# Attention's matmuls on four 64x64 tiles of TensorE, and each period's products in two halves

## The chip, the cores and the metric

The kernel runs on one core of one Trainium2 chip. The metric is the device time of one execution in microseconds; three executions are taken and their median is quoted.

## What is computed

Three layers follow one another. The first is attention inside chunks of 64 tokens, over 4 batches, 8 heads, 576 positions and 64 elements a head. The second is a gated layer from 512 to 1536 columns and back, the third a layer from 512 to 2048 and back with a rational function between. All arrays are float32.

```python
scores = scale * np.matmul(q_c, k_c.transpose(0, 1, 2, 4, 3))   # chunks of 64 by 64
attn = np.exp(scores - np.max(scores, axis=-1, keepdims=True))
attn = attn / (np.sum(attn, axis=-1, keepdims=True) + 1e-09)
x = np.matmul(attn, v_c)                  # then x becomes 2304 tokens by 512
x = ((x @ w_a) * (x @ w_b)) @ w_out
h = x @ w_in
g = (a0 + a1*h + a2*h*h + a3*h*h*h) / (1 + |b0|*|h| + |b1|*h*h + 1e-06)
out = g @ w_out2
```

## The kernel before

Every engine has its own hand-written program, and semaphores tie them together. The 2304 tokens are 18 units of 128 tokens, and 6 tiles of 384 tokens (3 units each). A unit holds two chunks (`cc`) and eight heads, which stand as four pairs (`r`) of two heads (`h`).

**Attention of a unit** passes five stages, one a period, so that five units are under way at once. In stage 0 TensorE (PE in the profile) transposes q and k (L515, four transposes each into the banks `QT` and `KT`) and ScalarE (ACT) copies them out (L823, L824). In stage 1 PE makes the scores: 16 matmuls of 64 rows by 64 columns with 64 moving columns (L539), all into the bank `SC`. They use two of the four 64x64 quarters of the array: head 0 has rows and columns 0 to 63, head 1 rows and columns 64 to 127. VectorE (DVE) takes the maximum (L1083) and subtracts it (L1085), ACT takes the exponential (L837), and DVE sums (L1090), adds 1e-9 (L1092), inverts (L1094) and multiplies (L1098). In stage 2 PE transposes the result into the bank `AT` (L515) and ACT copies it in two halves of 64 partitions into `attnT` (L832), whose off-diagonal blocks stay zero. In stage 3 PE multiplies with v: 8 matmuls of 128 rows by 64 columns with 128 moving columns (L557), half of which multiply the zeros, into the bank `XP`. ACT rounds x out of that bank (`x_hi`, L841) and DVE takes the rest (`x_lo`, L1076). The float32 matmuls of stages 1 and 3 are two records each in the trace, each with a weight load of its own; a transpose is one.

**The lead** is the first five units (`LEAD`), with transposes of the identity between the stages to keep PE busy. **The merged stage** follows: 15 periods, three to a tile for the first five tiles. Each has the attention stages of five units and then 24 matmuls with 384 moving columns. In the first two periods of a tile they are the products a and b of one step (`merged_block` with `r < G1`): ACT copies b out (L892), DVE multiplies a with it (L1112), ACT rounds that (`g_hi`, L894) and DVE takes the rest (`g_lo`, L1115). In the third period they are the four sums of the down product, which ACT copies out (L900). Late in the stage ACT also rounds operands for what comes next (`round_t` at L881, `round_w` at L863), two behind each of several periods, and GpSimd (POOL) makes the sums they come from. All that ACT and DVE do stands in one fixed order per engine: an instruction whose wait is not over holds up those behind it.

**The rest**, from 157.8 us on, is the gated layer's other columns (L643, L596) and the third layer.

The order of a period on PE before is: transposes of q; product with v; transposes of k; transposes of the attention of the unit before; scores; 24 products.

Of the kernel before, what the change touches and what calls it, by code (L numbers as in the profile page):

```python
# [20 lines left out]
def attention_moe_moe2(nc, q, k, v, w_a, w_b, w_out1, w_in, w_out2, a, b, out):  # L21
# [63 lines left out]
    with ExitStack() as ctx:  # L85
# [63 lines left out]
        attnT = tmp[:, 4 * D:6 * D].rearrange("p (r h n) -> p r h n", r=HP, h=2)  # L149

        def grouped(x):
            return x.rearrange("p (g k) -> p g k", k=CH)

        def spread(x):
            return x[:, 0:8].unsqueeze(2).to_broadcast([P, 8, CH])

        QT, KT, SC, AT, XP = range(3, 8)
# [240 lines left out]
        def _(pool):  # L398
            nc.gpsimd.memset(ident[:], 0.0).then_inc(consts_ready, 1)
            nc.gpsimd.memset(attnT, 0.0).then_inc(consts_ready, 1)  # L400
            nc.gpsimd.memset(bias_ln[:], QC * 2.0 ** -SHIFT).then_inc(consts_ready, 1)
            nc.gpsimd.memset(bias_exp[:], -SHIFT * math.log(2.0)).then_inc(consts_ready, 1)
            pool.wait_ge(consts_ready, 4)
# [103 lines left out]
        def _(pe):  # L507
# [10 lines left out]
            def attention(turn, slot, stages):  # L518
# [3 lines left out]
                lead = isinstance(i, int) and i < LEAD  # L522
# [5 lines left out]
                def wait_scores():  # L528
                    pe.wait_ge(qkT_copied, 2 * i)
                    if 2 in stages:  # L530
                        pe.wait_ge(sub_done, i - 1)

                def scores():
                    for r in range(HP):
                        for cc in range(2):
                            at = slice((2 * r + cc) * CH, (2 * r + cc + 1) * CH)
                            for h in range(2):
                                rows = slice(h * HD, (h + 1) * HD)
                                last = nc.tensor.matmul(ps[rows, SC, at], qT[rows, at], kT[rows, at], start=True, stop=True)  # L539
                    last.then_inc(scores_done, 1)  # L540

                def transpose_attn():
                    pe.wait_ge(attn_done, i - 1)
                    if 3 in stages:
                        pe.wait_ge(attnT_copied, 2 * (i - 2))
                    transposes(AT, attn).then_inc(attnT_done, 1)

                def times_v():
                    v_turn, v_slot = before(turn, slot, 3)
                    pe.wait_ge(attnT_copied, 2 * (i - 2))  # L550
# [26 lines left out]
                else:  # L577
# [3 lines left out]
                    if 3 in stages:  # L581
                        times_v()
                    if 0 in stages:
                        transposes(KT, qk_raw(slot)[1]).then_inc(qkT_done, 1)
                    if 1 in stages:
                        wait_scores()
                    if 2 in stages:
                        transpose_attn()
                    if 1 in stages:
                        scores()  # L590
# [18 lines left out]
            def first1(kk):  # L609

                t, f = kk // G1, kk % G1
                if kk == PLAIN:
                    pe.wait_ge(x_ready, UNITS)
                    pe.wait_ge(part_copied, DC * MERGED)
# [4 lines left out]
                tok = slice(t * TILE, (t + 1) * TILE)  # L619
                for m in range(2):  # L620
                    last = product3(ps[:, 2 * (kk % 2) + m, 0:TILE],
                                    [(w_cols(2 * m * PW + c * G1 * P + f * P), both(x_hi, x_lo, c, tok))
                                     for c in range(DC)])
# [70 lines left out]
            def merged_block(t, r, last=False):  # L694

                if r < G1:
                    if r == 0:
                        pe.wait_ge(x_ready, UPT * t + UPT)
                        pe.wait_ge(part_copied, DC * t + 1)
                    pe.wait_ge(product_done, G1 * t + r + 1)  # L700
                    tok = bass.ds(t * TILE, TILE)
                    for m in range(2):
                        last = product3(ps[:, m, 0:TILE],
                                        [(w_cols(2 * m * PW + c * G1 * P + r * P), both(x_hi, x_lo, c, tok))
                                         for c in range(DC)])
                    last.then_inc(ab_done, 1)
                else:
                    pe.wait_ge(w_ready, FIRSTS)
                    pe.wait_ge(g_ready, G1 * t + G1)
                    for c in range(DC):  # L710
                        if last and c == 2:
                            attention(*LAST, {3, 4})
                        if c in (0, DC - 1):
                            pe.wait_ge(part_copied, DC * t + (1 if c == 0 else 2))
                        product3(ps[:, (2, 0, 1, 2)[c], 0:TILE],
                                 [(w_cols(4 * PW + f * D + c * P), both(g_hi, g_lo, 1 + f))
                                  for f in range(G1)]).then_inc(part_done, 1)
# [52 lines left out]
            pe.wait_ge(consts_ready, 5)  # L770
# [8 lines left out]
            for r, stages in enumerate(({0, 1, 2, 3, 4}, {1, 2, 3, 4}, {2, 3, 4})):  # L779
# [543 lines left out]
```

## Time and profile before

| | before |
|---|---|
| median of 3 executions | 911.8 us (911.66 to 912.16) |
| profiled execution | 911.71 us, its span 909.9 us |
| PE busy | 898.4 us, 99% of the span |
| DVE, ACT, POOL busy | 673.1, 515.4, 364.9 us |
| granted clock of TensorE | full in all 40 slices |

The span runs from the first to the last instruction of the program; 1.8 us of the execution lie around it. A busy share is an average over the whole span, and the merged stage is 126 us of it, so that stage is read by itself below. The engines' lines are numbered by the code above.

### The profile page before, as it was taken

Reading aid. Unit: us, or ns where it says so; the run is one execution under the profiler, and the core shown is the slowest. Engines: PE = TensorE matmul, PEld = TensorE weight load, DVE = VectorE, ACT = ScalarE, POOL = GpSimd, SP = SyncE. Lnnn points to the kernel's source line nnn. Section 1 sums busy time; section 2 is a strip of 40 time slices with the busy share of each in tenths; the row PEclk is TensorE's granted clock in tenths of the full one; section 3 lists DMA queues with packets and bytes.
Section 4 is the critical chain, followed back from the end, with each engine's and each line's share of the span. In section 5 each row is a group of like instructions: output and inputs, shape, how many; then the busy total and the mean of one; then the engine's idle time right before and its main releaser. Section 6 shows DMA issues by size and latency. Waiting matters only on the chain.

```text
span 909.9 us, 14077 instructions
## 1 busy us (share of the span) xinstructions
PE 898.4 (99%) x5596; PEld 849.3 (93%) x5596; DVE 673.1 (74%) x874; ACT 515.4 (57%) x787; POOL 364.9 (40%) x302
## 2 busy tenths in 40 slices
PE   8999999899999999999999999999999999999998
PEld 8898999899999999999999998999999999999996
DVE  3657553666666667656565799997999999989987
ACT  4655674344444444445554587886667566666562
POOL 2109133577887778888976023210111011100000
PEclk9999999999999999999999999999999999999999
DMA  9865310222222222223211020002000200000102
GB/s 206 177 151 106 83 24 25 82 70 70 70 68 70 70 65 77 68 82 98 71 44 57 13 93 1 1 1 93 1 1 0 92 2 1 1 1 29 42 36 104
DMA packets 103234, 53.35 MB, mean 59 GB/s; under 512 B 58880, under 2 KB 94720, under 8 KB 103168
## 3 DMA queue, kind: packets, MB, share of 16 engines
q1 hardware_dynamic: 103168, 52.45, 21.6%
q8 instruction: 44, 0.72, 0.3%
q14 instruction: 22, 0.18, 0.1%
HBM read 47.71 MB, written 4.72 MB: 58 GB/s over the span
## 4 chain that ended last, share of the span: by engine, by line
PE 92%; DVE 4%; ACT 2%; issue 1%; POOL 0%; DVEq 0%; ACTq 0%; POOLq 0%
PE ps L596 40%; PE ps L643 23%; PE ps L764 19%; PE ps L515 3%; PE ps L539 2%; PE ps L557 2%; PE ps L511 1%; DVE tmp L1267 1%; DVE tmp L1273 1%; ACT w L1041 1%; PE ps L632 0%; ACT g_hi L1054 0%; ACT tmp L1027 0%; ACT tmp L1024 0%; DVE tmp L1263 0%
## 5 line engine op out<-in xcount | busy, mean ns | idle before, releaser
L596 PE MATMUL ps<-x_hi,w 128*128 128x384 f32 x960 | 255.3, 337 | 0.6 <-DVE tmp L1286 0.3
L596 PEld LDWEIGHTS ps<-x_hi,w 128*128 128x128 f32 x960 | 174.4, 188 | 3.6 <-DVE tmp L1286 0.7
L764 PE MATMUL ps<-w,g_hi 128*128 128x512 f32 x576 | 177.5, 391 | 0.0
L596 PE MATMUL ps<-x_lo,w 128*128 128x384 f32 x480 | 160.8, 335 | 0.0
L596 PE MATMUL ps<-g_hi,w 128*128 128x384 f32 x560 | 148.7, 335 | 1.0 <-issue 1.0
L439 POOL TENSOR_TENSOR w<-w 128x512 fp32r<-128x512 f32 x32 | 47.0, 1476 | 231.8 <-ACT w L876 231.8
L643 PE MATMUL ps<-x_hi,w 128*128 128x384 f32 x480 | 134.0, 334 | 1.5 <-DVE tmp L1150 1.5
L764 PEld LDWEIGHTS ps<-w,g_hi 128*128 128x128 f32 x576 | 107.4, 188 | 21.0 <-ACT g_hi L1054 0.4
L764 PE MATMUL ps<-w,g_lo 128*128 128x512 f32 x288 | 112.1, 392 | 0.0
L1140 DVE TENSOR_TENSOR y<-y,ps 128x384 f32<-128x384 f32 x120 | 65.6, 552 | 58.6 <-PE ps L596 58.6
L643 PE MATMUL ps<-w 128*128 128x384 f32 x540 | 103.4, 334 | 1.2 <-ACT ps L935 1.2
L596 PEld LDWEIGHTS ps<-g_hi,w 128*128 128x128 f32 x560 | 101.7, 188 | 1.8 <-issue 1.4
L955 ACT CAST g_hi<-tmp 128x384 fp32r<-128x384 f32 x60 | 30.8, 514 | 116.4 <-DVE tmp L1155 90.5
L643 PEld LDWEIGHTS ps<-w 128*128 128x128 f32 x540 | 94.4, 188 | 1.5 <-ACT ps L935 1.5
L596 PE MATMUL ps<-g_lo,w 128*128 128x384 f32 x280 | 93.6, 334 | 0.0
L596 PEld LDWEIGHTS ps<-x_lo,w 128*128 128x128 f32 x480 | 90.1, 188 | 1.7
L643 PEld LDWEIGHTS ps<-x_hi,w 128*128 128x128 f32 x480 | 87.8, 188 | 1.8 <-DVE tmp L1150 1.8
L429 POOL TENSOR_TENSOR w<-w 128x512 fp32r<-128x512 f32 (+1 forms) x48 | 72.5, 1538 | 20.8 <-ACT w L863 19.7
L643 PE MATMUL ps<-x_lo,w 128*128 128x384 f32 x240 | 80.2, 334 | 0.0
L1041 ACT ACTIVATE w<-tmp,bias_ln 128x768 f32<-128x768 f32 x48 | 45.1, 940 | 61.8 <-DVE tmp L1273 61.5
L1024 ACT ACTIVATE tmp<-ps 128x768 f32<-128x768 f32 x48 | 39.0, 813 | 65.6 <-PE ps L596 65.6
L1267 DVE SCALAR_TENSOR_TENSOR tmp<-tmp,coef 128x768 f32<-128x768 f32 x48 | 52.7, 1098 | 28.5 <-ACT tmp L1027 28.4
(113 smaller groups left out, 1590.7 us busy)
## 6 DMA issues: line engine op xcount, KB each, us to landing
w<-in_moe_w_out SPq DMA_DIRECT2D x32, 256.0 KB, 3.0
out<-y SPq DMA_DIRECT2D x18, 256.0 KB, 2.0
y<-in_q SPq DMA_DIRECT2D x16, 256.0 KB, 4.4
y<-in_k SPq DMA_DIRECT2D x16, 256.0 KB, 4.9
y<-in_v SPq DMA_DIRECT2D x16, 256.0 KB, 3.2
w<-in_moe_w_a SPq DMA_DIRECT2D x16, 256.0 KB, 3.0
w<-in_moe_w_b SPq DMA_DIRECT2D x16, 256.0 KB, 3.6
w<-in_moe_w_in SPq DMA_DIRECT2D x16, 256.0 KB, 3.9
```

The lines of the kernel that those rows point to most:

```text
L429: nc.gpsimd.tensor_tensor(w[:, w_slot(n), LO, at:to], raw_w(n, at, to), w[:, w_slot(n), HI, at:to], ALU.subtract).then_inc(ws_ready, 1)
L439: nc.gpsimd.tensor_tensor(w2_at(w, fp, LO, i), w2_at(w32, fp, LO, i), w2_at(w, fp, HI, i), ALU.subtract).then_inc(w2_ready, 1)
L515: last = nc.tensor.transpose(ps[:, bank, r * P:(r + 1) * P], x[:, r * P:(r + 1) * P], ident[:])
L539: last = nc.tensor.matmul(ps[rows, SC, at], qT[rows, at], kT[rows, at], start=True, stop=True)
L596: last = nc.tensor.matmul(dst, left, right, start=n == 0, stop=n == 3 * len(pairs) - 1)
L643: last = nc.tensor.matmul(ps[:, bank, 0:TILE], left, moving, start=i == 0 and not onto, stop=i == 5, skip_group_check=onto)
L764: last = nc.tensor.matmul(out_bank(n), left[:, 2 * (m % 2) + e, u * P:(u + 1) * P], w[:, slot2(fp), right, DC * HALF + e * D:DC * HALF + ( ...
L955: nc.scalar.copy(g_hi[:, 2 * ti + n % 2, :], corner[:, 2 * (n % 2) + 1 - ti, :]).then_inc(g_hi_done, 1)
L1024: nc.scalar.activation(habs, h, ACT.Abs).then_inc(habs_done, 1)
L1041: nc.scalar.activation(rec, den3[m % 2], ACT.Ln, scale=2.0 ** -SHIFT, bias=bias_ln[:, 0:1]).then_inc(ln_done, 1)
L1140: nc.vector.tensor_tensor(y[:, t, at], y[:, t, at], ps[:, 4 + c, 0:TILE], ALU.add).then_inc(y_added, 1)
L1267: nc.vector.scalar_tensor_tensor(out=den[cur], in0=den[cur], scalar=coef[:, 6:7], in1=habs, op0=ALU.add, op1=ALU.mult).then_inc(den_done, 1)
```

## The change

Scores and products with v both become 16 matmuls of 64 rows by 64 columns with 64 moving columns, spread over all four 64x64 quarters of the array. `attnT` no longer holds zeros, and ACT copies it at once (L895 of the changed kernel in place of two of L832). Scores and x share two banks: scores stand in the upper half of the columns of banks 6 and 7, x in the lower half (in the lead x stands in banks 1 and 2). For that sharing PE waits for `x_ready` ahead of the scores and for `sub_done` ahead of the product with v. A period on PE becomes: product with v; transposes of q and k; 12 products; scores; transposes of attention; 12 products. On DVE the product a times b moves in between the sum and the addition of 1e-9 of the attention. On ACT the copy of attention moves behind those of k and q, and the rounding of a product moves to the next period, behind that of x.

```diff
-        attnT = tmp[:, 4 * D:6 * D].rearrange("p (r h n) -> p r h n", r=HP, h=2)
+        attnT = tmp[:, 4 * D:5 * D].rearrange("p (r s n) -> p r s n", r=HP, s=2)
...
-        QT, KT, SC, AT, XP = range(3, 8)
+        QT, KT, AT, SC = 3, 4, 5, 6
+        raw_scores = ps[:, SC:SC + 2, D // 2:D].rearrange("p c (r k) -> p c r k", k=CH)
+        def x_bank(i):
+            return 1 if i < LEAD else SC
+        def raw_x(i):
+            return ps[:, x_bank(i):x_bank(i) + 2, 0:D // 2].rearrange("p c (r q) -> p r c q", q=CH)
...
                     if 2 in stages:
                         pe.wait_ge(sub_done, i - 1)
+                    if not lead:
+                        pe.wait_ge(x_ready, i - 2)
                 def scores():
...
                             for h in range(2):
-                                rows = slice(h * HD, (h + 1) * HD)
-                                last = nc.tensor.matmul(ps[rows, SC, at], qT[rows, at], kT[rows, at], start=True, stop=True)
+                                rows, half = slice(h * HD, (h + 1) * HD), h ^ cc
+                                to = slice(D // 2 + r * CH, D // 2 + (r + 1) * CH)
+                                last = nc.tensor.matmul(ps[half * CH:(half + 1) * CH, SC + cc, to],
+                                                        qT[rows, at], kT[rows, at], start=True, stop=True)
...
+                    if not lead:
+                        pe.wait_ge(sub_done, min(i - 1, UNITS))
                     vs = v_raw(v_slot)
                     for r in range(HP):
-                        for h in range(2):
-                            last = nc.tensor.matmul(ps[h * HD:(h + 1) * HD, XP, r * P:(r + 1) * P],
-                                                    vs[:, (2 * r + h) * HD:(2 * r + h + 1) * HD],
-                                                    attnT[:, r, h, :], start=True, stop=True)
+                        for cc in range(2):
+                            rows = slice(cc * CH, (cc + 1) * CH)
+                            for h in range(2):
+                                last = nc.tensor.matmul(ps[h * HD:(h + 1) * HD, x_bank(i) + cc, r * CH:(r + 1) * CH],
+                                                        vs[rows, (2 * r + h) * HD:(2 * r + h + 1) * HD],
+                                                        attnT[rows, r, h ^ cc, :], start=True, stop=True)
...
+            def first_half(t, f, m):
+                if m == 0:
+                    if f == 0:
+                        pe.wait_ge(x_hi_done, UPT * t + UPT)
+                        pe.wait_ge(part_copied, DC * t + 1)
+                    pe.wait_ge(product_done, G1 * t + f + 1)
+                    product_hi(ps[:, 0, 0:TILE], first_operands(t, f, 0))
+                    if f == 0:
+                        pe.wait_ge(x_ready, UPT * t + UPT)
+                    product_lo(ps[:, 0, 0:TILE], first_operands(t, f, 0))
+                else:
+                    product3(ps[:, 1, 0:TILE], first_operands(t, f, 1)).then_inc(ab_done, 1)
+            def part_half(t, cs):
+                if cs[0] == 0:
+                    pe.wait_ge(w_ready, FIRSTS)
+                for f in range(G1):
+                    pe.wait_ge(g_ready, G1 * t + f + 1)
+                    for c in cs:
+                        if f == 0 and c == 1:
+                            pe.wait_ge(product_done, G1 * (t + 1) + 1)
+                        part_sum(t, f, c)
...
             for j in range(MERGED // 2):
                 for r in range(2 * RING):
-                    attention(2 * j + (LEAD + r) // RING, (LEAD + r) % RING, {0, 1, 2, 3, 4})
-                    merged_block(2 * j + r // UPT, r % UPT)
+                    for half in range(2):
+                        attention(2 * j + (LEAD + r) // RING, (LEAD + r) % RING, {0, 1, 2, 3, 4}, half)
+                        merged_half(2 * j + r // UPT, r % UPT, half)
...
+            def merged(turn, slot, stages, t, r):
+                attention(turn, slot, stages, 0)
+                if r > 0:
+                    first_g(G1 * t + r - 1)
+                if r == G1:
+                    copy_part(t, 0)
+                    copy_part(t, 1)
+                attention(turn, slot, stages, 1)
                 if r < G1:
+                    copy_b(G1 * t + r)
+                elif t < MERGED - 1:
+                    copy_part(t, 2)
+                    copy_part(t, 3)
```

On PE, in the second period of a tile, the attention's instructions stood in one piece ahead of the products (`ident,y` is a transpose of q or k, `ident,tmp` one of attention; the 24 products are L596):

```order
L515 MATMUL ps<-ident,y 128x128 [waits qkT_copied,qk_loaded0]
L515 MATMUL ps<-ident,y 128x128 x3
L557 MATMUL ps<-tmp,y 64x128 [waits x_ready,v_loaded0,attnT_copied]
L557 MATMUL ps<-tmp,y 64x128 x7
L515 MATMUL ps<-ident,y 128x128 x4
L515 MATMUL ps<-ident,tmp 128x128 [waits attn_done,attnT_copied,sub_done,qkT_copied]
L515 MATMUL ps<-ident,tmp 128x128 x3
L539 MATMUL ps<-tmp 64x64 x16
L596 MATMUL ps<-x_hi,w 128x384 [waits product_done]
L596 MATMUL ps<-x_lo,w 128x384
```

Now they stand in two pieces, with twelve products behind each (the first twelve begin at L616, the second at L628; L580 is the product with v, L557 the scores):

```order
L580 MATMUL ps<-tmp,y 64x64 [waits x_ready,sub_done,v_loaded0,attnT_copied]
L580 MATMUL ps<-tmp,y 64x64 x15
L530 MATMUL ps<-ident,y 128x128 [waits qkT_copied,qk_loaded0]
L530 MATMUL ps<-ident,y 128x128 x7
L616 MATMUL ps<-x_hi,w 128x384 [waits product_done]
L617 MATMUL ps<-x_hi,w 128x384
...
L621 MATMUL ps<-x_lo,w 128x384 x4
L557 MATMUL ps<-tmp 64x64 [waits x_ready,sub_done,qkT_copied]
L557 MATMUL ps<-tmp 64x64 x15
L530 MATMUL ps<-ident,tmp 128x128 [waits attnT_copied,attn_done]
L530 MATMUL ps<-ident,tmp 128x128 x3
L628 MATMUL ps<-x_hi,w 128x384
...
L580 MATMUL ps<-tmp,y 64x64 [waits x_ready,sub_done,v_loaded1,attnT_copied]
```

The product with v has moved ahead of the transposes of q, the scores ahead of those of attention and behind twelve products, and both have a wait more (`sub_done`, `x_ready`).

On DVE, from the sum of the exponentials in the same kind of period to the rest of x, the order was:

```order
L1090 TENSOR_REDUCE ssum<-tmp 128x8 [waits exp_done]
L1092 TENSOR_SCALAR ssum<-ssum 128x8 [waits sum_done]
L1094 RECIPROCAL sinv<-ssum 128x8 [waits eps_done]
L1098 TENSOR_TENSOR tmp<-tmp,sinv 128x512 [waits attnT_done,inv_done]
L1112 TENSOR_TENSOR tmp<-ps,tmp 128x384 [waits b_copied]
L1115 TENSOR_TENSOR g_lo<-tmp,g_hi 128x384 [waits g_hi_done]
L1076 TENSOR_TENSOR x_lo<-ps,x_hi 128x4x128 [waits x_hi_done]
```

and it is now:

```order
L1166 TENSOR_REDUCE ssum<-tmp 128x8 [waits exp_done]
L1187 TENSOR_TENSOR tmp<-ps,tmp 128x384 [waits b_copied]
L1170 TENSOR_SCALAR ssum<-ssum 128x8 [waits sum_done]
L1172 RECIPROCAL sinv<-ssum 128x8 [waits eps_done]
L1176 TENSOR_TENSOR tmp<-tmp,sinv 128x2x4x64 [waits attnT_done,inv_done]
L1192 TENSOR_TENSOR g_lo<-tmp,g_hi 128x384 [waits g_hi_done]
L1153 TENSOR_TENSOR x_lo<-ps,x_hi 128x4x128 [waits x_hi_done]
```

The product of a and b (`tmp<-ps,tmp`) has moved ahead of three small instructions and of the multiplication that the transposes of attention wait for.

On ACT, around the two roundings of `round_t` behind the first of three periods (`w<-w`), the order was:

```order
L892 COPY tmp<-ps 128x384 [waits ab_done]
L894 CAST g_hi<-tmp 128x384 [waits product_done]
L881 CAST w<-w 128x768 [waits t_made] x2
L841 CAST x_hi<-ps 128x4x128 [waits av_done]
L832 COPY tmp<-ps 64x8x64 [waits av_done,attnT_done]
L832 COPY tmp<-ps 64x8x64
L823 COPY tmp<-ps 128x512 [waits scores_done,qkT_done]
```

and it is now:

```order
L953 COPY tmp<-ps 128x384 [waits ab_done]
L944 CAST w<-w 128x768 [waits t_made] x2
L903 CAST x_hi<-ps 128x4x128 [waits av_done]
L957 CAST g_hi<-tmp 128x384 [waits product_done]
L888 COPY tmp<-ps 128x512 [waits scores_done,qkT_done]
L889 COPY tmp<-ps 128x512
L895 COPY tmp<-ps 128x512 [waits av_done,attnT_done]
```

The roundings stood behind `g_hi`; they now stand ahead of it and of x's rounding, because `g_hi` has moved to the next period.

## Rows read from the trace of the kernel before

**Rows 1.** The page's table of engines: busy us, share, instructions.

```profile
PE 898.4 (99%) x5596; PEld 849.3 (93%) x5596; DVE 673.1 (74%) x874; ACT 515.4 (57%) x787; POOL 364.9 (40%) x302
```

**Rows 2.** Windows by stage: PE, PEld, DVE, ACT, POOL busy us, PEclk, DMA.

```profile
31.68:157.83 126.15, 124.73 (x1233) 115.38 (x1229) 70.49 (x123) 73.47 (x138) 40.29 (x30) 1.00 0.39 85
```

**Rows 3.** Timeline of PE, one period: start us, length us, line, form, records.

```profile
103.83 0.45 PE L596 MATMUL ps<-x_hi,w 128*128 128x384 f32 x1
104.11 0.34 PE L596 MATMUL ps<-x_lo,w 128*128 128x384 f32 x1
...
108.13 0.60 PE L515 MATMUL ps<-ident,y 128*128 128x128 f32 x4
108.66 1.09 PE L557 MATMUL ps<-tmp,y 128*64 128x128 f32 x16
109.68 0.66 PE L515 MATMUL ps<-ident,y 128*128 128x128 f32 x4
...
110.71 1.15 PE L539 MATMUL ps<-tmp 64*64 64x64 f32 x32
111.78 0.45 PE L596 MATMUL ps<-x_hi,w 128*128 128x384 f32 x1
```

**Rows 4.** Lines L539 and L557: duration ns min/median/max of one record.

```profile
L539 PE MATMUL ps<-tmp x576: 218/218/268, 10.8 to 134.7; 64*64 64x64 f32 x192
...
L557 PE MATMUL ps<-tmp,y x288: 272/273/323, 19.9 to 145.0; 128*64 128x128 f32 x144
```

**Rows 5.** PE and its loads, product with v to 68.40, scores to 70.42 us.

```profile
68.29 0.33 PE L557 MATMUL ps<-tmp,y 128*64 128x128 f32 x2
...
68.29 0.20 PEld L557 LDWEIGHTS ps<-tmp,y 128*64 128x64 f32 x4 [0.17 <-issue]
...
70.34 0.27 PE L539 MATMUL ps<-tmp 64*64 64x64 f32 x2
...
70.34 0.19 PEld L539 LDWEIGHTS ps<-tmp 64*64 64x64 f32 x4 [0.17 <-issue]
```

**Rows 6.** Timeline of ACT behind the products that end at 108.13 us.

```profile
108.33 0.48 ACT L892 COPY tmp<-ps 128x384 f32<-128x384 f32 x1 [2.30 <-PE ps L596]
109.43 0.51 ACT L894 CAST g_hi<-tmp 128x384 fp32r<-128x384 f32 x1 [0.62 <-DVE tmp L1112]
109.85 1.56 ACT L881 CAST w<-w 128x768 fp32r<-128x768 f32 x2
111.31 0.58 ACT L841 CAST x_hi<-ps 128x512 fp32r<-128x512 f32 x1
```

**Rows 7.** Timeline of DVE in the same stretch.

```profile
107.23 0.69 DVE L1098 TENSOR_TENSOR tmp<-tmp,sinv 128x512 f32<-128x512 f32 x1
108.84 0.56 DVE L1112 TENSOR_TENSOR tmp<-ps,tmp 128x384 f32<-128x384 f32 x1 [0.92 <-ACT tmp L892]
109.97 0.56 DVE L1115 TENSOR_TENSOR g_lo<-tmp,g_hi 128x384 fp32r<-128x384 f32 x1 [0.58 <-ACT g_hi L894]
111.92 0.69 DVE L1076 TENSOR_TENSOR x_lo<-ps,x_hi 128x512 fp32r<-128x512 f32 x1 [1.39 <-ACT x_hi L841]
```

**Rows 8.** Timeline of PE: the two places where it stands still.

```profile
78.36 0.63 PE L515 MATMUL ps<-ident,tmp 128*128 128x128 f32 x4 [0.43 <-DVE tmp L1098]
...
140.30 0.66 PE L515 MATMUL ps<-ident,tmp 128*128 128x128 f32 x4
141.94 0.41 PE L596 MATMUL ps<-g_hi,w 128*128 128x384 f32 x1 [0.99 <-issue]
```

**Rows 9.** Timeline of DVE ahead of the first of them.

```profile
75.96 2.14 DVE L1098 TENSOR_TENSOR tmp<-tmp,sinv 128x512 f32<-128x512 f32 x1
```

**Rows 10.** Timeline of ACT: roundings of weights behind the sums.

```profile
124.71 1.14 ACT L863 CAST w<-w 128x512 fp32r<-128x512 f32 x2
```

**Rows 11.** Timeline of PE in the lead.

```profile
18.77 1.15 PE L539 MATMUL ps<-tmp 64*64 64x64 f32 x32
19.85 1.09 PE L557 MATMUL ps<-tmp,y 128*64 128x128 f32 x16
```

More of the change, by code:

```diff
@@ L516, in transposes, with attention @@
                 return last
-            def attention(turn, slot, stages):
+            def attention(turn, slot, stages, part=0):
                 i = turn * RING + slot
-                lead = isinstance(i, int) and i < LEAD
+                lead = i < LEAD
                 def wait_qk():
@@ L618, in first1 @@
                     pe.wait_ge(product_done, kk)
-                tok = slice(t * TILE, (t + 1) * TILE)
                 for m in range(2):
-                    last = product3(ps[:, 2 * (kk % 2) + m, 0:TILE],
-                                    [(w_cols(2 * m * PW + c * G1 * P + f * P), both(x_hi, x_lo, c, tok))
-                                     for c in range(DC)])
+                    a_b = ps[:, 2 * (kk % 2) + m, 0:TILE]
+                    if kk == PLAIN:
+                        pe.wait_ge(part_copied, DC * MERGED - 1 + m)
+                        product_hi(a_b, first_operands(t, f, m))
+                        if m == 0:
+                            pe.wait_ge(x_ready, UNITS)
+                        last = product_lo(a_b, first_operands(t, f, m))
+                    else:
+                        last = product3(a_b, first_operands(t, f, m))
                 last.then_inc(ab_done, 1)
@@ L692, in second_sum @@
                               for fi in range(G1)]).then_inc(sum_done1, 1)
-            def merged_block(t, r, last=False):
-                if r < G1:
[L697 to L706, printed above, removed]
-                else:
[L708 to L717, printed above, removed]
@@ new lines, in first_operands @@
+            def first_operands(t, f, m):
+                return [(w_cols(2 * m * PW + c * G1 * P + f * P), both(x_hi, x_lo, c, slice(t * TILE, (t + 1) * TILE)))
+                        for c in range(DC)]
+            def first_half(t, f, m):
+                if m == 0:
+                    if f == 0:
[6 more added lines that the diff above has]
+                    product_lo(ps[:, 0, 0:TILE], first_operands(t, f, 0))
+                else:
+                    product3(ps[:, 1, 0:TILE], first_operands(t, f, 1)).then_inc(ab_done, 1)
@@ new lines, in part_bank, with part_sum @@
+            def part_bank(c):
+                return ps[:, (2, 0, 1, 2)[c], 0:TILE]
+            def part_sum(t, f, c):
+                if f == 0 and c in (0, DC - 1):
+                    pe.wait_ge(part_copied, DC * t + (1 if c == 0 else 2))
+                at = 4 * PW + f * D + c * P
+                for left, right in ((HI, g_hi), (LO, g_hi), (HI, g_lo)):
+                    last = nc.tensor.matmul(part_bank(c), first_w(left, at, P), right[:, 1 + f, :],
+                                            start=f == 0 and (left, right) == (HI, g_hi), stop=f == G1 - 1 and right is g_lo)
+                if f == G1 - 1:
+                    last.then_inc(part_done, 1)
@@ L809, in _, with attention @@
         def _(act):
-            def attention(turn, slot, stages):
+            def attention(turn, slot, stages, part=0):
                 i = turn * RING + slot
@@ L1068, in _, with attention @@
         def _(dve):
-            def attention(turn, slot, stages):
+            def attention(turn, slot, stages, s=None):
                 i = turn * RING + slot
-                lead = isinstance(i, int) and i < LEAD
+                lead = i < LEAD
                 def rest_x():
                     dve.wait_ge(x_hi_done, i - 2)
-                    at = bass.ds((i - 3) * P, P)
-                    nc.vector.tensor_tensor(x_lo[:, :, at], ps[:, XP, :].rearrange("p (c n) -> p c n", c=DC),
-                                            x_hi[:, :, at], ALU.subtract).then_inc(x_ready, 1)
+                    nc.vector.tensor_tensor(x_unit(x_lo, i - 3), raw_x(i), x_unit(x_hi, i - 3), ALU.subtract).then_inc(x_ready, 1)
                 if 3 in stages and not lead:
@@ L1103, in _, with product1 @@
             dve.wait_ge(part_copied, 1)
[L1104 to L1107 removed]
+            def product1(s, a_bank, slot, same_slot=False):
                 dve.wait_ge(b_copied, s + 1)
```

139 lines of the change are left out of this document (81 added, 58 removed).

## The prediction

> **What bounds the kernel now.** The page's table of engines comes first: PE is busy 99% of the span, its weight loads 93%, DVE 74%, ACT and POOL less [rows 1]. So time is won by taking work off PE and lost by making it wait, and the question is whether four quarters of the array do the same matmuls in less time than two. The change touches the lead and the merged stage alone. A window over the merged stage shows PE busy for 124.73 of 126.15 us, at full clock [rows 2]; busy PE is not PE at its peak, so I read one period in the timeline [rows 3]. It takes 111.78 - 103.83 = 7.95 us: 24 products 4.30, transposes of q 0.53, product with v 1.02, eight transposes 1.03, scores 1.07. These follow without a hole, and 13 of the 15 periods look like this. PE stands still at two places, for 0.43 us until DVE's L1098 is done, and at 141.94, where the sums wait for `g_lo` [rows 8]. The four transposes ahead of the second begin at 140.30 and need 0.5 as elsewhere, so that wait is 141.94 - 140.80 = 1.1 us. The first comes from one DVE instruction of 2.14 us [rows 9] that takes 0.69 elsewhere [rows 7].
>
> **What four tiles can give.** The trace has scores on two quarters, head 0 in one, head 1 in the diagonally opposite one, in turn. They share no rows and no columns. If quarters worked side by side, the two heads' matmuls would show it already. 16 scores are 32 records and the last is 0.218 long [rows 3, 4], so they start over 1.15 - 0.22 = 0.93 us, 0.058 per matmul of two records. The product with v has 16 records over 1.09 - 0.27 = 0.82 us; eight matmuls of 128 moving columns, at a pitch of 0.109. In the first 0.08 us of the scores (to 70.42) four weight loads have started, those of both heads, but only two matmul records, the two of one matmul; the other head's begin after it. In the first 0.11 us of the product with v (to 68.40) it is the same [rows 5]. So I find pairs of records of one matmul under way together and no overlap of one quarter with another. And 0.058 for 64 columns against 0.109 for 128 says that halving the moving columns just about halves the time: as the product with v also doubles its matmuls, from 8 to 16, it gains nothing. I take both groups at the pitch of the scores.
>
> The Trainium skill speaks for the change here: TensorEngine Tiling (Array Packing), section Key Properties, has different tiles load weights and multiply in parallel. By that rule each group would need half the slots; this trace's two quarters don't show it, so in the sum it has no place, but it is a rival.
>
> **The sum, part by part.**
> - Scores: the same 32 records of the same form, 0.
> - Product with v: 32 records as the scores', 1.07 to 1.08, in place of 1.02 [rows 3]: +0.054 for each of 18 units, +1.0. Bounds: -0.41 each if pairs overlap (below), and +0.2 each if neighbours on the same rows got in each other's way, as far as no row shows them.
> - Changes of shape: four in a period before and after. What differs is what stands behind the scores. Before, it is a product: the second follows the first after 0.28 us [rows 3], where (4.30 - 0.11) / 24 = 0.17 is usual, 0.11 lost. After, it is transposes, which behind the product with v take 0.66 for four instead of 0.60 [rows 3], 0.06 lost. 15 x -0.05 = -0.7. In the lead the product with v follows the scores 1.08 us after their start [rows 11], a change of shape between; afterwards both have one shape: -0.1 for two units and, as ACT copies attention at once and PE waits for that copy at the lead's end, some 0.1 more. I take -0.3; if q and k land too late for it, 0.
> - Waits that go: 0.43 and 1.1 [rows 8], -1.5. Their covers now are the twelve products ahead of the transposes of attention, and the half of the sums that needs only the first `g`.
> - Waits that come, since on ACT and DVE the order is other. Let Z be the end of a period's products on PE (108.13 in rows 3). ACT copies b at Z+0.20 for 0.48 [rows 6]. PE starts the product with v at Z+0.09, transposes from Z+1.17, and the first twelve matmuls at Z+2.10. Behind the copy of b ACT now has, in three periods, the two roundings of 0.83 with 0.73 from one start to the next [rows 6], before it comes to x and `g_hi`: x starts at Z + 0.20 + 0.39 + 2 x 0.73 = Z+2.05 (0.39 is the copy's 0.48 less the 0.09 by which neighbours overlap), `g_hi` at Z+2.54, done Z+3.05; `g_lo` on DVE, 0.56 [rows 7], done Z+3.65. If the next period is one of sums, PE needs it after six matmuls, Z + 2.10 + 6 x 0.173 = Z+3.14: wait 0.6. One period later ACT rounds two pieces of w in 1.14 [rows 10] between the sums' copies and x: x done Z + 0.20 + 0.39 + 1.06 + 0.58 = Z+2.23, seen at 2.30, wanted at 2.10: 0.2.
> - In the last two periods PE has no q and k to transpose and comes 0.93 earlier. Bank 0 must be free: copy of b, then the product a times b, 0.56 [rows 7], done at Z+1.30; PE is there at Z+1.17: 0.15. Then the scores wait for `x_ready`: with two roundings (0.73 and 0.53) x starts at Z+1.85, `g_hi` at 2.34, `g_lo` from 2.88, x_lo at 3.35 for 0.69 [rows 7], seen Z+4.1; PE is there at 1.33 + 2.19 + 0.09 = Z+3.6: 0.5. In the last period `g_lo` waits behind DVE's small instructions and the 0.69 of attention: product done Z+1.25, multiplication Z+2.3, `g_lo` Z+2.95 against PE at Z+2.3: 0.65. And while POOL works and DVE's instructions stretch as in [rows 9], I allow 0.3 once, ahead of the scores. Together 0.6 + 0.2 + 0.15 + 0.5 + 0.65 + 0.3 = +2.4.
>
> The order of the other periods costs nothing. Where ACT has no roundings, x is rounded once the product with v is done, by Z+1.85, and `g_lo` (Z+2.9) and x_lo (Z+3.5) come before the scores at Z + 2.10 + 2.08 + 0.09 = Z+4.27. That cover is 0.7 us thick, and what stands behind the scores would be late by whatever eats through it. SP's loads wait for the same semaphores at much the same times, and the rest of the kernel starts later by the sum.
>
> Sum: 1.0 - 0.7 - 0.3 - 1.5 + 2.4 = +0.9. The profiled execution took 911.71 us, its span of 909.9 and 1.8 around it, which is 0.1 below the median; on it the sum gives 912.6, on the median 912.7. I say **912.6 us**, no change that could be told: a measurement of this kernel can tell about 0.2%, 1.8 us, from none.
>
> **Rivals.**
> - *Quarters do work side by side*, because head 0 and head 1 both wrote the bank `SC` before and now matmuls that follow one another use two banks. The Trainium skill, same page, section Gotcha 1: PSUM Pressure, says that different row tiles can't access the same PSUM bank at the same time; no run here shows whether that is what kept them apart. Then 16 matmuls need 8 slots of 0.058: -0.47 for the scores and 1.02 - 0.61 = -0.41 for the product with v, -15.8 over 18 units. PE then comes 0.47 earlier to each of its waits: five waits grow by that and the sums of four tiles get one of 0.3, +3.5 beside the 0.9 of the other terms less the 1.0 for v. Result 911.7 - 15.8 + 3.5 - 0.1 = about 899; if only every second pair overlaps, about 904. For it: the pairs of records that do start together. Against: two banks don't help head 0 and head 1, which are neighbours and still share one. Chance 0.24.
> - *A dearer DVE chain, slower.* Product a times b now stands ahead of attention's last four steps, and the rest of x behind them must be done before the scores. It decides once copy of b to x_lo is longer than the cover of 0.7. One instruction stretched by 1.45 [rows 7, 9] costs 0.7. If four or five periods had one, +3 to +4: 916. POOL is busy 40.29 of 126.15 us of the stage [rows 2], and only one of these long ones shows before. Chance 0.09, with anything like it on the v matmuls.
> - *The new waits are smaller than worked out*, with the rest as forecast: 910.5 to 911.5, still no difference. It is part of the forecast's 0.67.
>
> **How the numbers follow.** Forecast with its own range of 911 to 914.5: 0.67. Of it I put 0.03 below 910.0 and 0.11 above 913.6, the bounds of 0.2%. With 0.24 for the first rival: faster 0.27. With 0.09 for the second: slower 0.21, and 0.52 for the same. Leaving out 2 in 10 takes the range down into the first rival: 900 to 915.
>
> **What would show it.** Right: 32 records of the product with v spread over 0.93 us, a period of 7.95, waits of about 0.6 at the sums near 118 us and again near 142, and about 0.5 ahead of the scores near 135. Wrong: records of either group closer than 0.029 on average, so a group shorter than 1 us and periods near 7.1 (first rival), or idle PE ahead of the scores in most periods behind `x_lo` (second). If the shape changes cost other than 0.05 a period, the end of the merged stage tells: it was 157.83 and should be 158.7.

## The result and the profile after

The changed kernel takes **920.11 us** (median of 5 runs, 917.85 to 922.66) against 911.8 before: ratio 1.0089, 95% interval 1.0076 to 1.0102. It is 0.9% slower, and outside the range of 900 to 915. The profiled execution is the slowest of the five, 922.66 us with a span of 919.6. The first product of the part behind the merged stage starts at 167.43 us, where it was 157.83: all of the loss is ahead of it.

The page's table of engines and its row of the granted clock, against [rows 1]:

```profile
PE 892.9 (97%) x5884; PEld 840.8 (91%) x5884; DVE 683.4 (74%) x874; ACT 502.9 (55%) x769; POOL 364.0 (40%) x301
...
PEclk9998989999999999999999999999999999999999
```

PE is busy 5.5 us less and its span is 9.7 longer, so it waits. One period in the timeline of PE, against [rows 3]:

```profile
101.18 0.42 PE L616 MATMUL ps<-x_hi,w 128*128 128x384 f32 x1
...
103.47 0.69 PE L557 MATMUL ps<-tmp 64*64 64x64 f32 x32
104.09 0.66 PE L530 MATMUL ps<-ident,tmp 128*128 128x128 f32 x4
...
106.78 0.69 PE L580 MATMUL ps<-tmp,y 64*64 64x64 f32 x32
107.40 1.09 PE L530 MATMUL ps<-ident,y 128*128 128x128 f32 x8
108.25 0.42 PE L616 MATMUL ps<-x_hi,w 128*128 128x384 f32 x1
```

The period is 108.25 - 101.18 = 7.07 us, where it was 7.95. The scores take 0.69 in place of 1.15 and the product with v 0.69 in place of 1.09; less the last record's 0.22, 32 records start over 0.47. The four quarters do give what the first rival said. Where it is lost again, the waits of PE over the merged stage tell (engine, line, what it waited for, us, times, longest):

```profile
PE ps L755 <- DVE g_lo L1192: 8.4, 3, 3.8
PE ps L557 <- DVE x_lo L1153: 5.3, 2, 2.8
PE ps L616 <- DVE tmp L1187: 0.5, 1, 0.5
PE ps L616 <- ACT x_hi L903: 0.4, 1, 0.4
```

Five waits of 1.5 to 3.8 us, each for the last instructions of DVE's chain. The groups of DVE in the same stretch (busy us, mean ns of one) show which of them is late:

```profile
L1176 DVE TENSOR_TENSOR tmp<-tmp,sinv 128x512 f32<-128x512 f32 x14 | 18.1, 1292 | 0.5
L1192 DVE TENSOR_TENSOR g_lo<-tmp,g_hi 128x384 fp32r<-128x384 f32 x10 | 11.4, 1136 | 0.0
...
L1166 DVE TENSOR_REDUCE ssum<-tmp 128x8 f32<-128x512 f32 x14 | 9.6, 686 | 10.6 <-ACT tmp L899 10.6
L1187 DVE TENSOR_TENSOR tmp<-ps,tmp 128x384 f32<-128x384 f32 x10 | 5.6, 558 | 6.2 <-ACT tmp L953 6.2
```

The multiplication (L1176) has a median of 0.69 and a longest of 2.27; `g_lo` (L1192) goes from 0.55 to 2.15. The sum over the exponentials (L1166) and the product of a and b (L1187) keep their 0.69 and 0.56. The timeline of all engines at the first stall names the partner:

```profile
64.39 1.83 POOL L460 TENSOR_TENSOR x_lo<-x_hi,x_lo 128x768 f32<-128x768 f32 x1 [32.44 <-PE ps L628]
...
65.34 0.91 DVE L1170 TENSOR_SCALAR ssum<-ssum 128x8 f32<-128x8 f32 x1
65.72 0.60 PE L755 MATMUL ps<-g_hi,w 128*128 128x384 f32 x2
...
66.30 1.81 POOL L462 TENSOR_TENSOR w<-x_lo,x_hi 128x768 f32<-128x768 f32 x1
66.34 0.52 PE L755 MATMUL ps<-g_hi,w 128*128 128x384 f32 x2
66.52 2.14 DVE L1176 TENSOR_TENSOR tmp<-tmp,sinv 128x512 f32<-128x512 f32 x1
66.69 0.34 PE L755 MATMUL ps<-g_lo,w 128*128 128x384 f32 x1
...
68.19 2.13 POOL L464 TENSOR_TENSOR w<-w,x_lo 128x768 f32<-128x768 f32 x1
68.58 2.15 DVE L1192 TENSOR_TENSOR g_lo<-tmp,g_hi 128x384 fp32r<-128x384 f32 x1
70.28 2.14 POOL L468 TENSOR_TENSOR w<-x_hi,x_lo 128x768 f32<-128x768 f32 x1
70.66 0.68 DVE L1153 TENSOR_TENSOR x_lo<-ps,x_hi 128x512 fp32r<-128x512 f32 x1
70.79 1.01 PE L755 MATMUL ps<-g_hi,w 128*128 128x384 f32 x2 [3.76 <-DVE g_lo L1192]
```

POOL's instruction ends at 66.30 + 1.81 = 68.11; the multiplication, 0.69 by itself, ends 0.55 later, so nearly all of its work comes behind POOL's. POOL's next one starts ahead of that end and takes 2.13 in place of 1.83, and `g_lo` waits for it in turn. `x_lo`, of which one input is in PSUM, starts beside a POOL instruction and takes its 0.68. The two that make PE late have both inputs in SBUF. This is what the Trainium skill states (SBUF — State Buffer, section Who interferes with whom): a DVE instruction with two SBUF inputs contends with a GpSimd (here POOL) instruction that reads SBUF, and the second to issue waits for all of the first. The trace agrees, but for the first 0.14 us of the multiplication's 0.69. Two inputs in SBUF are not the only case: the small addition of 1e-9 (L1170), with one input of 8 columns in SBUF, takes 0.91 here beside POOL's instruction of 64.39, and 0.16 elsewhere. What decides for that one no run separates.

A second loss stands behind the wait. Windows of the same trace (stretch, us, busy us of PE, PEld, DVE, ACT, POOL, then the granted clock):

```profile
31.00:66.00 35.00, 35.00 (x499) 31.54 (x498) 20.93 (x39) 18.84 (x37) 2.56 (x3) 1.00 0.69 155
66.00:70.80 4.80, 1.04 (x7) 0.71 (x5) 4.73 (x5) 0.00 (x1) 4.64 (x4) 0.88 0.72 164
70.80:75.00 4.20, 4.20 (x43) 3.65 (x44) 1.29 (x3) 1.69 (x4) 4.12 (x3) 0.50 0.00 0
75.00:77.90 2.90, 2.90 (x16) 2.65 (x15) 2.10 (x3) 1.79 (x4) 2.82 (x2) 0.74 0.00 0
```

PE was idle for 3.76 us, and for the 4.2 us behind it the granted clock is 0.50, the level of 1.2 GHz, and 0.74 on average in the 2.9 us after that: two products take 1.01 us where they took 0.60 at full clock (65.72 above).

### The profile page after: what moved, and what is told of

It is laid out like the page before. It is cut to its first block, busy times and chain, and to the rows that moved or that the text cites. A ratio compares the mean times of both kernels' runs of the same rounds, so it can differ in the third digit from the quotient of the medians.

```text
span 919.6 us, 14651 instructions
## 1 busy us (share of the span) xinstructions
PE 892.9 (97%) x5884; PEld 840.8 (91%) x5884; DVE 683.4 (74%) x874; ACT 502.9 (55%) x769; POOL 364.0 (40%) x301
## 4 chain that ended last, share of the span: by engine, by line
PE 86%; DVE 7%; ACT 3%; SPq 2%; issue 1%; DMA 1%; DVEq 0%; ACTq 0%
PE ps L628 35%; PE ps L679 23%; PE ps L821 19%; PE ps L530 2%; PE ps L755 2%; DVE tmp L1176 1%; SPq L313 1%; PE ps L557 1%; DVE tmp L1350 1%; DVE g_lo L1192 1%; PE ps L621 1%; PE ps L616 1%; DVE tmp L1356 1%; PE ps L617 1%; PE ps L580 1%
## 5 line engine op out<-in xcount | busy, mean ns | idle before, releaser
L628 PE MATMUL ps<-x_hi,w 128*128 128x384 f32 x864 | 232.5, 339 | 0.5 <-DVE tmp L1369 0.3
L628 PEld LDWEIGHTS ps<-x_hi,w 128*128 128x128 f32 x864 | 158.8, 190 | 2.9 <-DVE tmp L1369 0.7
L628 PE MATMUL ps<-x_lo,w 128*128 128x384 f32 x432 | 145.7, 337 | 0.0
L679 PE MATMUL ps<-x_hi,w 128*128 128x384 f32 x480 | 133.9, 334 | 1.4 <-DVE tmp L1232 1.4
L628 PE MATMUL ps<-g_hi,w 128*128 128x384 f32 x480 | 126.5, 334 | 0.0
L679 PEld LDWEIGHTS ps<-x_hi,w 128*128 128x128 f32 x480 | 87.7, 188 | 1.8 <-DVE tmp L1232 1.8
L628 PEld LDWEIGHTS ps<-g_hi,w 128*128 128x128 f32 x480 | 87.0, 188 | 0.0
L628 PEld LDWEIGHTS ps<-x_lo,w 128*128 128x128 f32 x432 | 82.0, 190 | 1.7
L679 PE MATMUL ps<-x_lo,w 128*128 128x384 f32 x240 | 80.2, 334 | 0.0
L628 PE MATMUL ps<-g_lo,w 128*128 128x384 f32 x240 | 80.2, 334 | 0.0
```

What stands on the lines that cost most here:

```text
L628: last = nc.tensor.matmul(dst, left, right, start=n == 0, stop=n == 3 * len(pairs) - 1)
L679: last = nc.tensor.matmul(ps[:, bank, 0:TILE], left, moving, start=i == 0 and not onto, stop=i == 5, skip_group_check=onto)
```

## The experiments

Theory: POOL's instructions hold up the multiplication and `g_lo`, PE waits for them, and its clock falls. Rivals: DVE's new patterns are dearer by themselves; or DVE's new order is what costs. Besides, two readings of the quarters stood against each other. In the texts on record experiment 2 is called e4_two_quarters, experiment 4 e6_gated, and the first run of experiment 8 e13_filled. An edit moves the line numbers below it, so rows are best matched by names: `tmp<-tmp,sinv` is the multiplication, `tmp<-ps,tmp` the product of a and b.

**1. Did two quarters overlap before?** In the kernel before, the scores of head 0 and head 1 in turn became all of head 0, then all of head 1:

```diff
-for r in range(HP):
-    for cc in range(2):
-        for h in range(2):
+for h in range(2):
+    for r in range(HP):
+        for cc in range(2):
```

> The kernel before with its scores in another order: all eight of head 0, then all eight of head 1, in place of the two heads in turn. Theory (the two quarters did work side by side before): matmuls of one head follow each other at 0.116 (two records of 0.058) and have no partner, so 32 records take about 1.8 to 1.9 us in place of 0.93, and the time grows by 18 times 0.9: about 928. My reading in the prediction (no overlap of one quarter with another): 0.93 us as before and 911.8. Between the two if the queue of PE lets the second head's matmuls overtake.

Measured: 924.04 us, ratio 1.0131 (1.0116 to 1.0147). A row of its timeline:

```profile
42.71 1.90 PE L539 MATMUL ps<-tmp 64*64 64x64 f32 x32
```

1.90 less 0.22 is 1.68 us, where the heads in turn took 0.93. So the two diagonal quarters did work side by side before, and my reading in the prediction falls. One quarter alone takes 1.68 / 31 = 0.054 us per record, two at once 0.93 / 31 = 0.030, and four 0.015. The run is 12.2 us longer than the kernel before, near 18 x 0.75 = 13.5; I had expected 16. Both heads write the bank `SC` there, so one bank did not keep them apart either, as the first rival had it.

**2. Quarters, or banks?** In the changed kernel, the scores go to two quarters but still to two banks:

```diff
-rows, half = slice(h * HD, (h + 1) * HD), h ^ cc
+rows, half = slice(h * HD, (h + 1) * HD), h
```

> The changed kernel, but the scores of both half chunks of a head go to one column half: head 0 always on the first quarter, head 1 always on the diagonally opposite one, still in two banks; scores of the second half chunks so stand in the wrong rows, and the output is another. Theory (each quarter takes 0.058 us per record of its own, and quarters run side by side, in the kernel before too): 32 records on two quarters take 0.93 us from first to last start as in the kernel before, and the time grows by 17 times 0.45, less what waits hide: 924 to 928. Rival (it was the shared bank that kept the heads apart before; two banks let neighbours overlap): 0.48 us as in the changed kernel, 918 to 921.

Measured: 926.34 us, ratio 1.016 (1.0145 to 1.0175), 6.2 over the changed kernel. From its timeline:

```profile
38.68 1.15 PE L557 MATMUL ps<-tmp 64*64 64x64 f32 x32
```

1.15 again, as in [rows 3]: on two quarters a second bank gives nothing. No run has four quarters in one bank, so whether the 0.69 needs both banks stays open.

**3. The roundings that start POOL.** ACT rounds a piece, then POOL subtracts. The change put these roundings between the copy of b and the rounding of x; here they stand behind `g_hi` of the next period:

```diff
 def merged(turn, slot, stages, t, r, roundings=()):
     attention(turn, slot, stages, 0)
     if r > 0:
         first_g(G1 * t + r - 1)
+    for step, *which in roundings:
+        step(*which)
```

> The changed kernel with ACT's roundings of the pieces of t and w, after which POOL subtracts, put behind the rounding of g of the next period in place of between the copy of b and the rounding of x. Theory (DVE's instructions that read two SBUF operands are held up for as long as a POOL instruction runs): POOL's subtractions of the periods from 107 us on start when g_lo is done, so L1176 and L1192 keep 0.69 and 0.55 there in place of 2.27 and 2.15, and PE's waits of 3.1, 3.3, 2.8 and 1.7 us at 113, 121, 144 and 151 go, with the slow stretches behind them; the three collisions between 65 and 80 us stay. Some 11 to 14 us less than the changed kernel: 906 to 910. Rival (the long DVE instructions come from their new patterns or their new order): L1176 and L1192 stay long, 918 to 921.

Measured: 905.37 us, ratio 0.9925 (0.9908 to 0.9942), 14.7 less than the changed kernel and 0.6 below my range. Waits of PE in the merged stage:

```profile
PE ps L755 <- DVE g_lo L1184: 4.5, 2, 3.8
PE ps L616 <- DVE tmp L1179: 0.5, 1, 0.5
PE ps L621 <- DVE x_lo L1145: 0.2, 1, 0.2
```

The wait of 3.8 near 65 us stays, where POOL makes t; of the other four one of 0.7 is left (4.5 less 3.8). DVE's forms and order are those of the changed kernel, so neither makes the long instructions by itself.

**4. All of POOL's work kept out of the way.** The same, and POOL waits for `x_lo` of a period, then does two large instructions or four small ones:

```diff
+def behind_x_lo(period):
+    pool.wait_ge(x_ready, period + 3)
...
+behind_x_lo(5)
 make_t1(0)
 make_t2(0)
+behind_x_lo(8)
 make_t4(0)
```

> As the kernel with the roundings behind g, and POOL's eight large and eight small instructions for t and for the sums of w wait in addition for x_lo of a period, two large ones or four small ones in each, so that none runs beside the multiplication L1176 or g_lo L1192. Theory of the collisions: all L1176 last 0.69 and all L1192 0.55, no wait of PE over 1 us between 31 us and the end of the merged stage, a period of 7.07 to 7.32 throughout, and 20 us less than the changed kernel: 899 to 903, about where the first rival of the prediction had it. Rival (new patterns or order of DVE): no difference, 918 to 921. If POOL now comes too late for the weights, a wait at the first products behind the stage tells.

Measured: **899.0 us**, ratio 0.9858 (0.9843 to 0.9872), 21.1 less than the changed kernel. Groups of DVE:

```profile
L1184 DVE TENSOR_TENSOR tmp<-tmp,sinv 128x512 f32<-128x512 f32 x14 | 9.7, 692 | 0.5
...
L1200 DVE TENSOR_TENSOR g_lo<-tmp,g_hi 128x384 fp32r<-128x384 f32 x12 | 6.7, 560 | 1.2 <-ACT g_hi L1013 1.2
```

and waits of PE in the merged stage:

```profile
PE ps L771 <- DVE g_lo L1200: 0.7, 1, 0.7
PE ps L632 <- DVE tmp L1195: 0.5, 1, 0.5
```

Every multiplication takes 0.69 again. Nothing behind the stage came late.

**5. The same work, put back in the way.** Only what POOL waits for differs from experiment 4:

```diff
-    pool.wait_ge(x_ready, period + 3)
+    if period < 14:
+        pool.wait_ge(eps_done, period + 5)
+    else:
+        pool.wait_ge(x_ready, period + 3)
```

> The kernel with POOL's waits (e6_gated), but POOL waits for the step ahead of the reciprocal of a period's attention (eps_done) in place of x_lo: the same POOL work, the same number in each period, the same order of ACT and PE, started 0.4 us ahead of the multiplication. Theory: in the periods with two large POOL instructions the multiplication takes about 2.2 and g_lo, or x_lo's turn behind it, comes 3 us late; PE waits for 2 to 4 us in three or four of them, with a slow stretch behind each: 910 to 918. Rival (something else in the changed place of the roundings or waits made e6_gated fast): 898 to 901, all L1176 0.69.

Measured: 918.68 us, ratio 1.0067 (1.0051 to 1.0084), 19.7 over experiment 4 and 0.7 over my upper bound: which semaphore POOL waits for is enough to make such a loss. Its timeline also gives the price by size; first POOL's small pieces, then the large ones:

```profile
109.94 0.74 POOL L438 TENSOR_TENSOR w<-w 128x256 f32<-128x256 f32 x1 [4.50 <-DVE ssum L1181]
...
110.13 1.09 DVE L1187 TENSOR_TENSOR tmp<-tmp,sinv 128x512 f32<-128x512 f32 x1
...
110.76 1.07 POOL L440 TENSOR_TENSOR w<-w 128x256 f32<-128x256 f32 x1
```

```profile
90.33 1.83 POOL L482 TENSOR_TENSOR w<-w 128x768 f32<-128x768 f32 x1 [7.41 <-DVE ssum L1181]
...
90.45 2.25 DVE L1187 TENSOR_TENSOR tmp<-tmp,sinv 128x512 f32<-128x512 f32 x1
```

Beside 256 columns of POOL (0.74 us) the multiplication takes 1.09, beside 768 (1.83) 2.25: what is left of POOL's instruction (0.55 and 1.71), and then 0.54 of its own 0.69.

**6. DVE's order undone.** The product of a and b goes back behind the multiplication; POOL and ACT as changed:

```diff
-                    if s is not None:
-                        product1(s, 0, 0, s % G1 == 1)
                     dve.wait_ge(sum_done, i)
...
                     if first is not None:
+                        product1(first, 0, 0, first % G1 == 1)
                         rest_g1(first, 0, 1 + r % UPT)
```

> The changed kernel with DVE's product of a and b put back behind attention's last four steps, as before the change; POOL and ACT as changed. Theory (POOL's instructions collide with L1176 and g_lo wherever they meet): POOL works without a pause from 64 us on and for two instructions at the four later places, so g_lo or the multiplication still meets it; the long ones move a little and few go: 916 to 921. Rival (the changed order of DVE made the multiplication and g_lo neighbours and is what costs; the prediction's second rival in its own words): the stalls shrink to the 0.4 of the kernel before at most, 903 to 908.

Measured: 911.92 us, ratio 0.9999 (0.9989 to 1.0008). I missed this: it is 8.2 less than the changed kernel and neither theory's number. The instructions of DVE now lie elsewhere against POOL's; multiplications of 2.12 and 2.17 us and a `g_lo` of 1.04 are left between 67 and 82 us, and the longest behind 100 is a `g_lo` of 0.87. PE's waits in the merged stage still add up to 10.4 us, in place of 14.6.

**7. The same order without collisions.** Experiment 4 with the edit of experiment 6:

> e6_gated with DVE's product of a and b behind attention's last four steps. With no collisions the order of DVE should matter little: g_lo ends as it did or 0.4 us later, and PE waits for the product at one or two places for up to 1 us more: 899 to 902. If the order has a price or a gain of its own it shows here, clean of POOL.

Measured: 903.55 us, ratio 0.9912 (0.9897 to 0.9926), 4.6 over experiment 4 and 1.6 over my bound. Waits of PE in the merged stage:

```profile
PE ps L632 <- DVE tmp L1193: 2.5, 5, 1.3
PE ps L771 <- DVE g_lo L1198: 1.7, 5, 0.4
PE ps L771 <- DVE tmp L1193: 0.5, 1, 0.5
```

So with POOL out of the way DVE's changed order is worth 4.6 us; with POOL as changed it costs 8.2. The same edit has two signs, and where POOL runs decides.

**8. What the clock costs.** Transposes of the identity fill the waits of the changed kernel and shorten none:

```diff
 for f in range(G1):
+    if f == 1 and cs[0] == 0:
+        keep_warm({1: 32, 3: 28, 4: 12}.get(t, 0), AT)
     pe.wait_ge(g_ready, G1 * t + f + 1)
...
+keep_warm({LEAD + 9: 26, LEAD + 13: 24}.get(i, 0), AT)
 pe.wait_ge(x_ready, i - 2)
```

> The changed kernel with transposes of the identity into the bank of transposed attention, whose copy is made by then, ahead of five of the waits: 32, 28 and 12 ahead of the sums' waits for g_lo near 66, 120 and 150 us, 26 and 24 ahead of the scores' waits near 110 and 141. Nothing is waited for less, but PE is busy up to near the end of each wait. Theory (each long wait is followed by 3 to 6 us at half clock, which costs 1.2 to 2 us of its own): products behind them start 0.173 apart, no longer 0.28 to 0.47, and five places give 1.2 to 1.7 each: 912 to 915. Rival (the stretched steps are late operands): still stretched, 919 to 922.

Measured: 919.39 us, ratio 1.0075 (1.006 to 1.009). I had put one group a period too early: where PE had no wait 26 transposes took 2.9 us, and the wait near 113 us stayed open. With `LEAD + 10`:

> As e13_filled, with the fourth group of transposes at the right place: ahead of the scores' wait of 2.8 us near 113 us in place of one period earlier, where PE had nothing to wait for and lost 2.9 us to them. In the trace of e13_filled the products behind the filled waits start 0.173 apart, those behind the one left open (115 us) 0.28 to 0.47. So five waits as long as in the changed kernel, and no stretched stretch behind them: 1.5 to 2.1 us less for each of the four long ones, some 6 to 7 less than the changed kernel in all, 913 to 915. If it gives 917 or more, the half clock cost less than its stretched rows say, since other waits take up what it frees.

Measured: 914.17 us, ratio 1.0029 (1.0019 to 1.0039), 5.9 less than the changed kernel. PE at the first stall:

```profile
65.05 3.65 PE L526 MATMUL ps<-ident 128*128 128x128 f32 x32
69.00 0.62 PE L756 MATMUL ps<-g_hi,w 128*128 128x384 f32 x2 [0.30 <-DVE g_lo L1195]
69.45 0.34 PE L756 MATMUL ps<-g_lo,w 128*128 128x384 f32 x1
```

Two products take 0.62 behind the wait, where they took 1.01, and the granted clock stays 1.00 here:

```profile
71.00:75.00 4.00, 4.00 (x56) 3.68 (x57) 3.09 (x6) 3.62 (x7) 3.92 (x3) 1.00 0.01 4
```

**9. Did the kernel before pay for POOL too?** POOL's waits of experiment 4 in the kernel before:

> The kernel before with POOL's waits for x_lo alone, as in e6_gated, ACT unchanged. Its trace shows one multiplication of 2.14 us with a wait of 0.4 on PE behind it and no other wait from POOL, so I expect 911.2 to 911.7, nothing that can be told: POOL's timing matters only with the changed order of DVE and ACT. If it gives over 2 us, the kernel before paid for collisions too and the comparison of e6_gated with it is not one of the change.

Measured: 912.06 us, ratio 1.0002 (0.9994 to 1.0011), the same as the kernel before. It did not; what experiment 4 gains over the kernel before, 12.8 us, is the change's own.

**10. The size of the quarters' gain.** Experiment 4 with the edit of experiment 2:

> e6_gated with the scores on two quarters, as in e4_two_quarters (scores of the second half chunks stand in the wrong rows). With no collisions to hide it, 18 groups of scores cost 0.45 each more, 8.1 in all, less 0.5 for each unit of the lead that waits for its data anyway: 906 to 907. It is the size of what four quarters give the scores.

Measured: 905.38 us, ratio 0.993 (0.9917 to 0.9944), 6.4 over experiment 4. The merged stage has 14 groups of scores, and 14 x 0.45 = 6.3: the four of the lead are not seen in the sum.

**11. Two more steps put forward.**

> e6_gated with two steps put forward: in the lead's last unit ACT copies the transposed attention ahead of the exponential (PE waited 1.2 us for that copy), and in the last period with a product DVE does g_lo ahead of the multiplication (PE waited 0.8 us for g_lo). 0.5 and 0.3 to 0.7 us less: about 898, at the edge of what can be told from e6_gated.

Measured: 898.96 us, ratio 0.9859 (0.9844 to 0.9874), the same as experiment 4 within what can be told. The wait for `g_lo` fell from 0.7 to 0.5; in the lead q and k landed later in the profiled run, so the other step's worth stays open.

## Why the prediction was wrong

Two steps failed, in opposite directions: the quarters gave far more than the sum has, and the waits that came took more than that back.

**What four tiles can give: wrong.** This step said that no quarter overlaps another, from the first records of [rows 5]. Experiments 1 and 2 showed the opposite. The first records of a group can't tell; the records per quarter against the length of the whole group do. The 0.058 per matmul was the joint pace of two quarters: one alone needs 2 x 0.054 = 0.11. In place of 0 for the scores and +1.0 for the product with v, each gives: -0.45 and -0.40 a period, and the period is 7.95 - 0.45 - 0.40 = 7.10, measured 7.07. The comparison of 0.058 for 64 columns with 0.109 for 128 set the joint pace of two quarters beside that of matmuls of another shape, whose own overlap no run shows, so it said nothing of quarters. The Trainium skill's rule (TensorEngine Tiling (Array Packing), section Key Properties), which I had left out of the sum, holds here: 0.93 us on two quarters against 1.68 on one.

**Waits that go: half right.** The 0.43 [rows 8] is gone. At the place of the 1.1, the last tile's sums, PE still waits for `g_lo`: 1.5 in the changed kernel and 0.7 in experiment 4, which is the 0.65 that I had put there as a new wait.

**Waits that come: mis-sized by far.** I had 2.4 us; the trace has 8.4 + 5.3 + 0.5 + 0.4 = 14.6 us of waits in the merged stage, and the clock behind them. The places near 118 and 142 were named, and the row of the multiplication that takes 2.14 [rows 9] was in my hands, but I gave POOL one term of 0.3. I took the stretch as a chance event, and didn't look up what ran beside it. Nor was it the only one, as the second rival says: five instructions of DVE are stretched by more than 0.2 us in the kernel before, all between 74 and 88 us; the first and the last of them are

```profile
74.37 1.31 DVE L1092 TENSOR_SCALAR ssum<-ssum 128x8 f32<-128x8 f32 x1
...
86.12 1.12 DVE L1115 TENSOR_TENSOR g_lo<-tmp,g_hi 128x384 fp32r<-128x384 f32 x1 [0.58 <-ACT g_hi L894]
```

where the usual is 0.17 and 0.56. The timeline of POOL in the kernel before:

```profile
75.74 1.82 POOL L455 TENSOR_TENSOR w<-w 128x768 f32<-128x768 f32 x1
...
110.75 3.63 POOL L468 TENSOR_TENSOR w<-w 128x768 fp32r<-128x768 f32 x2 [20.73 <-ACT w L881]
```

The first is the partner of the multiplication of 2.14. The second shows why none is stretched behind 88 us: the roundings stood behind `g_hi` [rows 6], so POOL began at 110.75, when `g_lo` was done [rows 7]. I had followed these same roundings to their new place and priced them on ACT alone, and not what they release on POOL. The second rival had the right mechanism (a dearer chain on DVE), but one stretch a period for 0.7 us of it, where two neighbours stretch by 1.5 each.

**The clock: missing.** No step of mine had a wait change the pace of what follows. By experiment 8 it is 5.9 us.

**The sum as it was.** The change without collisions gives -12.8 (experiment 4). From there to the changed kernel it is +21.1, of which 14.7 at the places that the moved roundings set (experiment 3) and the other 6.4 where POOL makes t; 5.9 of the 21.1 is the clock. That -12.8 and +21.1 make the measured +8.3 is no check, since both are differences to experiment 4. Nor are all 21.1 shown to be POOL's: ACT's roundings also stand elsewhere in experiment 4, and no run makes POOL wait with the roundings where the change put them. In the changed kernel DVE never stood idle ahead of `g_lo` (the 0.0 in its row), and PE waited for ACT itself once, for 0.4 us, so ACT hardly set the time there; what its lateness would cost without the collisions, for which I had 0.6 + 0.2 + 0.5, stays open. The first rival's 899 is met by experiment 4 in part by luck: it counted 3.5 us of waits on top of my 2.4, and the merged stage there has 1.2. My chances were also added up 0.01 off: slower is 0.11 + 0.09 = 0.20, and the same 0.53.

## What to carry to other kernels

When a step is moved, follow what it releases on every engine, POOL too, and lay those instructions beside the ones of DVE that read two operands from SBUF (and, in these traces, its small addition); a stretched instruction in the trace before is a question of what ran beside it, not noise. To learn whether tiles of the array overlap, put their matmuls apart and compare whole groups. And a change that loses may hold one that wins: here waits on POOL, with the roundings moved, turn +0.9% into -1.4%.

## What the runs showed of the hardware

- Collisions cost both sides: POOL's 768 columns take 2.13 to 2.25 us when DVE is ahead, 1.83 alone.
- A reduction of one SBUF operand (0.69) and a subtraction or product with one operand in PSUM (0.68, 0.56) keep their times beside POOL's instructions in these traces. An addition of a constant to 8 columns in SBUF does not: 0.16 becomes 0.91 in the changed kernel, 0.17 becomes 1.31 in the kernel before.
- 32 records of 64 columns start over 1.68 us on one quarter after the other, 0.93 on two and 0.47 on four.
- In the changed kernel a wait of 3.76 us was followed by 4.2 us at a granted clock of 0.50. In the kernel before, after its wait of 1.1 us, the clock stayed 1.00:

```profile
142.00:146.00 4.00, 4.00 (x32) 3.58 (x33) 0.74 (x2) 2.86 (x6) 1.13 (x1) 1.00 0.00 0
```
